# Giving the block-transposed decay matrices of a linear-attention kernel VectorE slots of their own

## What is computed

```python
# attention: B, H, S, D = 4, 8, 768, 48
for t in range(S):
    cur = einsum('bhd,bhe->bhde', u * k[t], v[t])
    y[:, :, t] = einsum('bhd,bhde->bhe', r[t], state + cur)
    state = w[t][..., None] * state + einsum('bhd,bhe->bhde', k[t], v[t])
# x: 3072 tokens x 384
h = x @ w_in                      # 384 x 2048
x = maximum(0.01 * h, h) @ w_out  # 2048 x 384
# router: cosine of x and 8 expert vectors, / tau, softmax, argmax
# out[token] = gate * (relu(x @ w1[e]) @ w2[e])   # 384 x 1024 x 384
```

## Time and profile before

| what | value |
|---|---|
| median of 3 runs | 837.47 us (836.99 to 837.52) |
| the profiled execution | 837.12 us, span 835.2 us |
| TensorE matmul, weight load | 97%, 92% of the span |
| VectorE, ScalarE, GpSimd | 68%, 53%, 25% |
| granted TensorE clock | 1.00 over the span |
| first feed-forward layer, n = 0 to 127 | from 32.5 us to about 552 us |

### The profile page before, as it was taken

How to read it: one execution, slowest core, us unless ns; L and a number is a source line. 1 busy time by engine, 2 the same in 40 slices (tenths; PEclk the granted TensorE clock), 3 DMA queues, 4 the chain that set the end, 5 groups by cost and what they waited for, 6 DMA issues and landing times.

```text
span 835.2 us, 18049 instructions
## 1 busy us (share of the span) xinstructions
PE 814.3 (97%) x5633; PEld 764.3 (92%) x5633; DVE 571.3 (68%) x1315; ACT 439.1 (53%) x924; POOL 205.5 (25%) x286
## 2 busy tenths in 40 slices
PE   6999999999999999999999999999999999999997
PEld 5899999999989999999999999999989999898896
DVE  6889699789889788979878865636361512545563
ACT  5676464364464465455446435654563533555563
POOL 5611111121103012112112001212353322424433
PEclk9999999999999999999999999999999999999999
DMA  9976233145233123223221000513531512475392
GB/s 205 201 163 144 35 68 58 34 85 85 42 68 44 26 37 66 51 37 67 55 35 39 1 16 30 171 38 112 191 124 39 186 47 80 153 257 188 104 306 75
DMA packets 165306, 78.55 MB, mean 94 GB/s; under 512 B 135486, under 2 KB 153253, under 8 KB 165090
## 3 DMA queue, kind: packets, MB, share of 16 engines
q1 hardware_dynamic: 156402, 64.81, 31.8%
q0 software_dynamic: 4544, 10.85, 4.0%
q10 hardware_dynamic: 4272, 1.82, 1.0%
HBM read 112.90 MB, written 11.63 MB: 149 GB/s over the span
## 4 chain that ended last, share of the span: by engine, by line
PE 80%; DVE 8%; issue 4%; ACT 3%; DMA 1%; ACTq 0%; SPq 0%; DVEq 0%; POOL 0%; POOLq 0%
PE bank L1058 20%; PE bank L1037 19%; PE bank L1110 13%; PE bank L1146 13%; PE bank L963 3%; PE bank L1127 3%; PE bank L991 2%; PE bank L986 2%; PE bank L930 2%; DVE Fi L1639 1%; PE bank L971 1%; DVE Xi L1655 1%; PE bank L1092 1%; DVE gl L1726 1%; PE bank L1000 1%
## 5 line engine op out<-in xcount | busy, mean ns | idle before, releaser
L1037 PE MATMUL bank<-xhl,WRh 128*128 128x384 f32 x768 | 218.9, 339 | 0.2 <-issue 0.2
L1037 PEld LDWEIGHTS bank<-xhl,WRh 128*128 128x128 f32 x768 | 141.2, 188 | 0.4 <-issue 0.4
L1058 PE MATMUL bank<-WRh,gh 128*128 128x384 f32 x384 | 135.8, 354 | 0.0
L1404 ACT COPY gw<-bank 128x384 f32<-128x384 f32 x128 | 61.5, 480 | 132.3 <-PE bank L1037 132.2
L1037 PE MATMUL bank<-xhl,WRl 128*128 128x384 f32 x384 | 130.0, 339 | 0.0
L1058 PE MATMUL bank<-WRh,gl 128*128 128x384 f32 x384 | 129.8, 338 | 0.0
L1058 PE MATMUL bank<-WRl,gh 128*128 128x384 f32 x384 | 129.7, 338 | 0.0
L1410 ACT CAST gh<-gw 128x384 fp32r<-128x384 f32 x128 | 65.5, 512 | 97.3 <-DVE gw L1719 82.9
L1719 DVE SCALAR_TENSOR_TENSOR gw<-gw 128x384 f32<-128x384 f32 x128 | 72.6, 567 | 50.5 <-ACT gw L1404 50.3
L1726 DVE TENSOR_TENSOR gl<-gw,gh 128x384 fp32r<-128x384 f32 x128 | 79.0, 617 | 34.0 <-ACT gh L1410 29.5
L1894 DVE TENSOR_TENSOR hl<-bank,hh 128x512 fp32r<-128x512 f32 x56 | 36.1, 686 | 84.6 <-ACT hh L1445 84.2
(11 more groups left out here) (199 smaller groups left out, 1644.7 us busy)
## 6 DMA issues: line engine op xcount, KB each, us to landing
stage<-in_moe_w_dram SPq DMA_DIRECT2D x96, 768.0 KB
Kn<-in_k_dram SPq DMA_DIRECT2D x24, 192.0 KB, 3.5
Vn<-in_v_dram SPq DMA_DIRECT2D x24, 192.0 KB, 3.6
x_moe<-x2s SPq DMA_DIRECT2D x24, 192.0 KB, 3.0
Rn<-in_r_dram SPq DMA_DIRECT2D x21, 192.0 KB, 2.8
wraw<-in_moe_w_out_dram SPq DMA_DIRECT2D x4, 768.0 KB, 7.5
eraw<-in_moe_w_dram SPq DMA_DIRECT2D x4, 768.0 KB, 9.0
Wn<-in_w_dram SPq DMA_DIRECT2D x152, 16.0 KB, 1.8
```

Of the source, the lines that this page charges most:

```text
L1037: mm = pe.matmul(bank[F_BANK[n % 2]][:, 0:GN], win(t_)[:, f // 4, k_, cols], xhl[G % 2][:, a, k_, :], start=(k_ == 0 and n_ == 0), stop=(k ...
L1058: mm = pe.matmul(bank[O_BANK[i]][:, 0:DM], a[:, z, cols], wout(t_)[:, f, :], start=(f == 0 and n_ == 0), stop=(f == FT - 1 and n_ == 2))
L1404: act.copy(gw[:, n % 2, :], bank[F_BANK[n % 2]][:, 0:GN]).then_inc(s_g0, 1)
```

## The change

Chunks m >= 5 get three offsets of their own on VectorE (`BLOCK_SLOTS`): turn, `decay_to`, `decay_from`. For i = 0, 1, 2 they are (-5, -3, -2), (0, 2, 4), (6, 8, 9). The turn stands behind `leak` of its stage, each scan part ahead of `leak` of its own. `next_w`, ScalarE's check and the router's products are placed by them.

```diff
--- before.py
+++ after.py
@@ -256,16 +256,23 @@
             return bank[bk][:].rearrange("p (h t) -> p h t", h=HP)
 
         turn_w_at, turn_at, score_at, sum_at = {}, {}, {}, {}
+        block_at, decay_to_at, decay_from_at = {}, {}, {}
+        BLOCK_SLOTS = ((-5, -3, -2), (0, 2, 4), (6, 8, 9))
         FIRST_SLOTS = ((-1, -1, 1, 3), (3, 4, 6, 8), (8, 9, 11, 13))
         SLOTS = ((-2, -1, 1, 3), (3, 4, 6, 8), (8, 9, 11, 13))
         for m_ in range(GT, NC):
             g_, i_ = divmod(m_, GT)
             turn_w_at[m_], turn_at[m_], score_at[m_], sum_at[m_] = [
                 FT * (g_ - 1) + x for x in (FIRST_SLOTS if g_ == 1 else SLOTS)[i_]]
+            block_at[m_], decay_to_at[m_], decay_from_at[m_] = [FT * (g_ - 1) + x for x in BLOCK_SLOTS[i_]]
 
         def at(table, n):
 
             return [m for m in range(GT, NC) if table[m] == n]
+
+        def blocks(table, n):
+
+            return [m for m in range(BLOCKED, NC) if table[m] == n]
 
 
         moves = x2s[:, 2, 0:KT * HEAD_PAD].rearrange("p (k c) -> p k c", k=KT)
@@ -606,11 +613,10 @@
                                 fill(m // GT)
                             if m + NSLOT < NC:
                                 next_v(m + NSLOT)
-                            if m % GT == GT - 1 and m + 2 < NC:
+                        for m in blocks(block_at, n - 3):
+                            if m + 2 < NC:
                                 next_w(m + 2)
                         for m in at(turn_w_at, n - 4):
-                            if m % GT < GT - 1 and m + 2 < NC:
-                                next_w(m + 2)
                             if m + NSLOT < NC:
                                 next_load(m + NSLOT)
                     elif f == 0 and 0 < G < NG:
@@ -640,11 +646,12 @@
                         fill(m // GT)
                     if m + NSLOT < NC:
                         next_v(m + NSLOT)
-                    if m % GT == GT - 1 and m + 2 < NC:
+                if n == turn_w_at[GT + 1] + 4:
+                    next_w(GT + 3)
+                for m in blocks(block_at, n - 3):
+                    if m + 2 < NC:
                         next_w(m + 2)
                 for m in at(turn_w_at, n - 4):
-                    if GT < m and m % GT < GT - 1 and m + 2 < NC:
-                        next_w(m + 2)
                     if m + NSLOT < NC:
                         next_load(m + NSLOT)
                 if n == 2 * FT + 4:
@@ -1269,7 +1276,7 @@
 
             def check_slot(m):
 
-                return turn_w_at.get(m, -3) + 3
+                return block_at[m] + 1 if m >= BLOCKED else turn_w_at.get(m, -3) + 3
 
             def check_decays(m):
 
@@ -1492,8 +1499,9 @@
                             diagonal(m)
                         if n % 4 > 1 and n // 4 + 1 < NQ:
                             split_hi(2 * (n // 4) + n % 4)
-                        for m in at(turn_w_at, n - 3):
-                            check_decays(m)
+                        for m in range(GT, NC):
+                            if check_slot(m) == n:
+                                check_decays(m)
                     if not first and n == FT + 3:
                         act.wait_ge(s_en, E)
                         act.activation(ec[:, 1, :], ec[:, 0, :], ACT.Sqrt).then_inc(s_en, 1)
@@ -1923,11 +1931,16 @@
                             if turn_at[m] > turn_w_at[m]:
                                 decay_rk(m)
                         for m in at(turn_w_at, n - 1):
-                            if m > GT:
+                            if GT < m < BLOCKED:
                                 decay_to(m)
-                            decay_from(m)
+                            if m < BLOCKED:
+                                decay_from(m)
                             if turn_at[m] == turn_w_at[m]:
                                 decay_rk(m)
+                        for m in blocks(decay_to_at, n):
+                            decay_to(m)
+                        for m in blocks(decay_from_at, n):
+                            decay_from(m)
                     elif G < NG and f == 0:
                         x_lo(G)
                     if not first and n == SECOND - 1:
@@ -1937,9 +1950,9 @@
                         leak(n)
                     if not first:
                         for m in at(turn_w_at, n):
-                            if m >= BLOCKED:
-                                turn_w(m)
                             bonus_sum(m)
+                        for m in blocks(block_at, n):
+                            turn_w(m)
                         if n % 4 > 1 and n // 4 + 1 < NQ:
                             split_lo(2 * (n // 4) + n % 4)
                         if FT <= n < FT + 3:
@@ -1959,7 +1972,7 @@
                         have = 0
                     if 0 < G < NG - 1 and f >= (LAG + 1 if G == 1 else LAG):
                         light = not any(at(t_, n - 1) for t_ in (turn_at, score_at, sum_at))
-                        some = 0 if at(turn_w_at, n - 1) or (f == 3 and G > 1) else 3 if light else 2
+                        some = 0 if f in (4, 9, 14) or (f == 3 and G > 1) else 3 if light and f != 8 else 2
                         if f == FT - 1:
                             some = GT * E
                         products(first, G - 1, have, have + some)
```

## The result

The changed kernel took 834.23 us (median of 6 runs, 832.58 to 834.89), the kernel before 837.50 us in the same comparison (836.99 to 838.0). The ratio is 0.9958, with a 95% interval of 0.9945 to 0.9971: 3.3 us less. The forecast was 835.0 us and 0.3% less, in a range of 832.4 to 838.2.

The account below looks back on a forecast made before the run. TensorE, busy 97% of the span, bounds the kernel, so only its waits cost time. Removed 5.3 us of waits for Kt, added 2.8, net -2.5: 837.1 profiled to 834.6, expected median 835.0 us, range 832.4 to 838.2.

Parts of the forecast that it names:

- scans of the first block of a group: i = 0 scans moved from f = 15 to 13 and 14, into VectorE's idle time; saves 4.6 us at f = 1.
- n = 20: No route or idle time there, so scan-to at f = 2 delays Sx and y_lo in full: 0.7 us added.
- n = 52 and 84: Routed groups beginning a new batch element, where TensorE already waits at f = 4: 0.3 us added each.
- n = 36, 68, 100: Routed groups without a new batch element, 0.18 us spare before the k transposes: 0.12 us added each.
- n = 7 to 9: After the stalled first turn: 0.9 us new wait for the mask, 0.2 more at the k transposes.
- the first block-turned w: m = 5's turn, n = 8 to 6, waits for loads until 61.0 us; late mask costs 0.9 us, then 0.2.
- n = 111: Three products (1.4 us) stand before gl(111), which TensorE needs a stage and a half later: 0.
- the fills: SyncE's and ScalarE's fills follow a later y_lo, landing about 4 us after it; covered by 2 us.
- the check of w: ScalarE's check moves from f = 1, 6, 11 to 12, 1, 7; delays at f = 12 and 14 counted covered.
- Case 1: Rival: the queue at f = 2 to 4 and n = 6 has more give; 832.2 us, chance 0.12.
- case 3: Rival: Kt stays late at f = 1 by its own 2.9 us chain, only costs left; 840.3 us, chance 0.05.
- Case 2: Rival: the stall moves from f = 1 to f = 4, 0.5 us more per routed group; 837.4 us, chance 0.18.
- Case 4: Rival: GpSimd's products hold gl(68) back at f = 5, Kt 1.2 us late in five groups; 841 us, chance 0.07.

Follow-up runs that it names:

- Run 1: Changed kernel with the first block of a group (i = 0) back in its old slots, router's products as before: 837.36 us in one run.
- run 9: Only i = 0 gets the new slots; i = 1 and i = 2, m = 5 among them, keep the old ones: 832.50 us, ratio 0.9936.
- Run 4: Changed kernel with the scan-to of i = 1 at f = 1 instead of f = 2: 830.99 us, ratio 0.9919.
- run 2: Changed kernel with only m = 5 back in its old slots (turn at n = 8, both scans at n = 9): 833.04 us, ratio 0.9949.
- run 3: Changed kernel with VectorE forming the weights' low half before it turns w, in stages that have both: 833.48 us, ratio 0.9947.
- run 11: Changed kernel with i = 1's scan-to at f = 1, the low half ahead of the turn, and no router product at f = 2: 830.21 us, ratio 0.9912.
- run 8: Changed kernel with the router's dot products placed as before, slots as changed: 835.12 us in one run.
- run 6: Changed kernel with all of i = 1 back in its old slots (turn at f = 3, both scans at f = 4): 835.93 us in one run.
- run 7: Changed kernel with i = 1 in its old slots and its check of w put back to f = 6: 834.95 us in one run.
- run 10: Changed kernel with i = 1's scan-to at f = 1 and the weights' low half ahead of the turn: 830.41 us, ratio 0.9920.

## Why the prediction was right, and where it was not

**The bound and the gain.** TensorE's waits were the only thing to win, and all those for Kt went: 5.54 us by the stages for the 5.3 forecast. Run 1 brings them back in part, run 9 shows that the slots of i = 0 alone remove the 4.7 at f = 1. The step "scans of the first block of a group" holds: Kt is 2.1 us ahead of need where I said some 3. I had the leak follow its copy (it does so in five groups; at n = 79 a stretched gl(78) holds it 0.4 us), but left out that the cast behind it stands behind ScalarE's diagonal in every group. The 3 was the cover for the gain, so nothing was lost by it.

**The costs.** Forecast 2.8, measured 2.4. n = 20: 0.7 forecast, 0.67 measured. n = 52 and 84: 0.3 each, 0.24 measured. n = 36, 68, 100: 0.12 each, and that is what came. The mechanism was the forecast one: in n = 68 Sx starts 0.26 us later in its stage than before, where I took 0.3. n = 7 to 9: 0.9 and 0.2, measured 0.73 and 0.19. Run 4 shows for the f = 4 stages that it was the scan-to between mask and leak; run 2 shows that the rest is all m = 5.

**The step that failed** is in "the first block-turned w": "TensorE wants it at 64.47 (sums of m = 4)". I followed the queue behind the stalled turn to the mask and asked only who waits for that. Two instructions nearer, the low half of the weights has a consumer of its own, feature(8), wanted at 62.6 us. I priced that instruction as queue time and never asked who waits for it. That this term came out near, 0.9 for 0.73, is in part luck: the loss is the same 3.3 us of standing still, less about the same slack, whichever consumer meets it first. As advice it would have misled: getting the mask alone ahead of the turn would leave feature(8) where it is (not run), while the low half ahead of the turn, with the mask still behind it, cures it (runs 3 and 11).

**Zeros that held**: the products (run 8), n = 111, the fills, the moved loads (in the changed kernel no wait of TensorE is for a DMA between 30 and 490 us). **A zero that I argued too lightly**: the check of w. At f = 12, 1 and 7 it is free; run 6 shows that at f = 4 it costs 0.5 to 0.8 us in three of the groups (n = 38 with 40, 70, 102; against run 7). For i = 1 it costs nothing in the changed kernel because it goes with the turn to f = 1, and not to f = 4.

**The rivals.** Case 1 (all 5.3 kept) and case 3 (f = 1 not cured) are out. Case 2, 0.5 us more at f = 4 in each of the five routed groups than forecast, is out too: the forecast had 1.7 us at f = 4 and 1.5 came, and from gl(65) to Sx there are 8.53 us where there were 8.30, not 0.5 more. Case 4 did not come either: gl(68) starts before GpSimd's product in the changed kernel and keeps its length,

```profile
318.85 0.56 DVE L1734 TENSOR_TENSOR gl<-gw,gh 128x384 fp32r<-128x384 f32 x1 [1.41 <-issue]
...
319.58 1.04 POOL L753 TENSOR_TENSOR rku<-Rn,Kn 128x384 f32<-128x384 f32 x1
```

while at n = 79 GpSimd's product runs from 359.24 to 360.24, and gl, begun at 359.32, takes 1.34 us. The Trainium skill, page "SBUF — State Buffer", section "Who interferes with whom", has it that the one that starts first keeps the shared port to its end; the row at n = 79 agrees, while at n = 68 gl ends (319.41) before the product starts, and so tests nothing. The place where gl is stretched is one with time to spare, and the only one: 1 of 95 gl takes over 0.6 us in the changed kernel from 95 to 490 us, against 10 of 94 before.

## What to carry to other kernels

Of every instruction in the queue behind one that may wait for a DMA, ask who waits for it and when, and put the ones with the earliest consumer ahead of the wait. Move work to where its engine is idle because another sets the pace (here ahead of the low half that ScalarE delays), not merely to a stage with less in it: one stage later the same scan cost 2.7 us. And a large reordering should be tried in thirds: here one third gave 4.7 us, the others took 2.4 back and gave 0.8.

## What the runs showed of the hardware that I had not expected

At each undisturbed start of the scores, where the weight tiles go from 128 rows to 64, the weight loads idle for 0.25 us: 4.6 us over 18 stages, the same in the changed kernel and in the six experiments without a wait for Kt (runs 2, 3, 4, 8, 10, 11). No reordering on VectorE touched it. That the change of shape makes it is not shown, since no run keeps the shape.

A scan of VectorE's that starts while a product of GpSimd's (r, k and u, L753 and L756, about 1.0 us each) runs takes 1.15 to 1.23 us; every other scan takes 0.39 to 0.48. From 95 to 490 us 14 scans of 144 are so stretched in the kernel before and 12 of 136 in the changed one. The mean of a group of VectorE's instructions, 95 to 490 us, in the kernel before:

```profile
L1726 DVE TENSOR_TENSOR gl<-gw,gh 128x384 fp32r<-128x384 f32 x94 | 59.6, 634 | 19.9 <-ACT gh L1410 17.1 <-issue 1.7 <-PE bank L1058 0.7
...
L1639 DVE TENSOR_TENSOR_SCAN Fi<-Wn,floor 128x128 f32<-128x128 f32 x72 | 36.1, 559 | 0.0
L1655 DVE TENSOR_TENSOR_SCAN Xi<-Wn,Xi,floor 128x127 f32<-128x127 f32 x72 | 28.9, 463 | 0.0
```

and in the changed one:

```profile
L1734 DVE TENSOR_TENSOR gl<-gw,gh 128x384 fp32r<-128x384 f32 x95 | 53.6, 565 | 41.7 <-ACT gh L1417 39.2 <-issue 1.4 <-DVE slot L1815 1.1
L1663 DVE TENSOR_TENSOR_SCAN Xi<-Wn,Xi,floor 128x127 f32<-128x127 f32 x68 | 36.0, 590 | 0.0
...
L1647 DVE TENSOR_TENSOR_SCAN Fi<-Wn,floor 128x128 f32<-128x128 f32 x68 | 23.2, 405 | 0.0
```

The forward scans fell from 559 to 405 ns and the reversed ones rose from 463 to 590; an undisturbed one takes about 393 and 457. In the kernel before all the stretched scans are forward ones, 12 of the 14 at n = 20 and at f = 9, where both scan parts stood; in the changed kernel scan-to has left, and the 12 are reversed ones at the same places. What this costs is not shown by a run of its own.
